# Another formula for the first feed-forward's activation: arctan, two squares and a cubic in place of a second tanh with correction steps

## The reference

```python
# attention: per head, state = f*state + k v^T, y = q.state, f = sigmoid(f_logit)   (4 x 8 heads, 768 steps, dim 48)
x = y as [3072 tokens, 384]
# first feed-forward, d_ff = 2048
h  = x @ w_in
sp = log1p(exp(h))                    # softplus
g  = h * tanh(sp)
x  = g @ w_out
# second feed-forward, d_ff = 1536
out = (sigmoid(x @ w_gate) * (x @ w_val)) @ w_out2
```

## Time and profile before

| what | value |
|---|---|
| median of 3 runs | 1093.04 us (1092.76 to 1094.50) |
| span of the profiled execution, first to last instruction | 1088.3 us |
| median less span: what lies around the instructions | 4.7 us |
| TensorE busy | 1023.6 us (94%) |
| VectorE busy | 671.0 us (62%) |
| ScalarE busy | 571.5 us (53%) |
| GpSimd busy | 137.2 us (13%) |
| mean granted TensorE clock | 0.989 |

### The profile page before, as it was taken

The page is one execution under the profiler, slowest core; times in us unless marked ns, Lnnn a source line. Parts: engine busy times, 40 slices in busy tenths (PEclk is TensorE's granted clock), DMA queues, the critical chain, the costliest instruction groups (busy, mean ns, idle before and its releaser), DMA issues.

```text
span 1088.3 us, 14401 instructions
## 1 busy us (share of the span) xinstructions
PE 1023.6 (94%) x4765; PEld 826.9 (76%) x4765; DVE 671.0 (62%) x1035; ACT 571.5 (53%) x1067; POOL 137.2 (13%) x147
## 2 busy tenths in 40 slices
PE   4999998899999999988898789999999999999997
PEld 3777777688887888876676668888888888888885
DVE  7999997699998999989999942222222222222221
ACT  5677775688887888876767632221222112321222
POOL 2222222500000000004554440000000000000000
PEclk9999999899999999999999999999999999999999
DMA  5544441200000000001111110000000000100001
GB/s 145 147 139 137 130 145 53 58 1 1 1 1 1 1 0 0 0 1 44 44 37 36 44 37 1 1 1 1 30 29 0 0 0 0 58 1 1 1 1 58
DMA packets 35345, 37.58 MB, mean 35 GB/s; under 512 B 4064, under 2 KB 26080, under 8 KB 35296
## 3 DMA queue, kind: packets, MB, share of 16 engines
q1 hardware_dynamic: 35296, 36.98, 11.3%
HBM read 32.24 MB, written 4.72 MB: 34 GB/s over the span
## 4 chain that ended last, share of the span: by engine, by line
PE 66%; DVE 23%; issue 5%; ACT 4%; DVEq 1%; DMA 0%; SPq 0%; ACTq 0%
PE bank L834 21%; PE bank L836 21%; PE bank L835 20%; DVE sets L697 3%; DVE sets L702 3%; DVE sets L699 3%; DVE glo L706 3%; DVE sets L690 2%; DVE sets L689 2%; DVE prefix L570 2%; ACT qt L410 1%; DVE probs L597 1%; PE bank L777 1%; PE bank L754 1%; DVE state L614 1%
## 5 line engine op out<-in xcount | busy, mean ns | idle before, releaser
L834 PE MATMUL bank<-xhi,whi 128*128 (+1 forms) x720 | 286.4, 398 | 5.3 <-ACT prod L515 3.7
L836 PE MATMUL bank<-xhi,wlo 128*128 (+1 forms) x720 | 284.5, 395 | 0.0
L835 PE MATMUL bank<-xlo,whi 128*128 (+1 forms) x720 | 282.7, 393 | 0.0
L734 DVE TENSOR_TENSOR prod<-prod,bank 128x512 f32<-128x512 f32 x72 | 49.5, 688 | 293.7 <-PE bank L836 292.7
L834 PE MATMUL bank<-ghi,whi 128*128 128x512 f32 x504 | 201.9, 401 | 29.0 <-DVE glo L706 28.8
L836 PE MATMUL bank<-ghi,wlo 128*128 128x512 f32 x504 | 199.0, 395 | 0.0
L835 PE MATMUL bank<-glo,whi 128*128 128x512 f32 x504 | 198.3, 393 | 0.0
L834 PEld LDWEIGHTS bank<-xhi,whi 128*128 128x128 f32 x720 | 136.4, 189 | 35.5 <-issue 4.4
L836 PEld LDWEIGHTS bank<-xhi,wlo 128*128 128x128 f32 x720 | 136.4, 189 | 32.2
L835 PEld LDWEIGHTS bank<-xlo,whi 128*128 128x128 f32 x720 | 136.6, 190 | 30.9
L515 ACT ACTIVATE prod<-bank 128x512 f32<-128x512 f32 x72 | 43.1, 598 | 189.6 <-PE bank L836 189.5
(11 more groups left out here) (75 smaller groups left out, 1269.9 us busy)
## 6 DMA issues: line engine op xcount, KB each, us to landing
raw<-w_out_dram SPq DMA_DIRECT2D x28, 192.0 KB, 2.4
xb<-f_dram SPq DMA_DIRECT2D x48, 96.0 KB, 2.4
kb<-k_dram SPq DMA_DIRECT2D x48, 96.0 KB, 2.2
qb<-q_dram SPq DMA_DIRECT2D x48, 96.0 KB, 2.2
vb<-v_dram SPq DMA_DIRECT2D x24, 192.0 KB, 2.4
out_dram<-rows_out SPq DMA_DIRECT2D x18, 256.0 KB, 2.1
raw<-w_in_dram SPq DMA_DIRECT2D x16, 192.0 KB, 2.7
raw<-w_gate_dram SPq DMA_DIRECT2D x12, 192.0 KB, 2.5
```

Of the source, the lines that this page charges most:

```text
L734: dve.tensor_tensor(prod[:, i % NSET], prod[:, i % NSET], h_ps[1][:, :], ALU.mult).then_inc(p_done, 1)
L834: pe.matmul(ps, hi, xh, start=first, stop=False)
L835: pe.matmul(ps, hi, xl, start=False, stop=False)
L836: return pe.matmul(ps, lo, xh, start=False, stop=last)
```

## The change

The activation is computed by another formula. With t = tanh(h/2), it takes a = arctan(0.5 - 0.5 t), y = (2·ROOT·a - ROOT·pi/4)², z = (y - Y_SHIFT)², and g = (MISH_K - (z + Z_SHIFT)·y)·(t + 1)·h. ScalarE does `start` (one tanh from PSUM), `angle` (arctan), `square`, `shifted` (a second square) and `high`: five instructions a unit. VectorE does `silu` ((t + 1)·h, which now reads `h` from PSUM and frees the bank), `cubic`, `finish` and `low`: four a unit. The semaphore that frees the PSUM bank is `silu_done` in place of `act_h`. The order of the functions within an iteration is another one on both engines.

```diff
-                act.activation(st[:, 0], h_ps[i % 2][:, :], ACT.Tanh, scale=0.5).then_inc(wsl_done, 1)
-                act.activation(st[:, 1], h_ps[i % 2][:, :], ACT.Silu).then_inc(act_h, 1)
+                act.activation(st[:, 0], h_ps[i % 2][:, :], ACT.Tanh, scale=0.5).then_inc(tanh_done, 1)

-            def seed(p, i):
-                act.wait_ge(wsl_done, p * N1 + i + 1)
-                act.activation(st[:, 2], st[:, 0], ACT.Square, scale=-0.5, bias=half_bias).then_inc(sqx_done, 1)
-                act.activation(st[:, 3], st[:, 0], ACT.Tanh, scale=0.5 * SEED_B, bias=seed_bias).then_inc(f0_done, 1)
-            def error2(p, i):
-                act.wait_ge(a_done, p * N1 + i + 1)
-                act.activation(st[:, 0], st[:, 2], ACT.Square, scale=-SEED_A, bias=one_bias).then_inc(sq_done, 1)
+            def angle(p, i):
+                act.wait_ge(tanh_done, p * N1 + i + 1)
+                act.activation(st[:, 2], st[:, 0], ACT.Arctan, scale=-0.5, bias=half_bias).then_inc(angle_done, 1)
+            def square(p, i):
+                act.wait_ge(angle_done, p * N1 + i + 1)
+                act.activation(st[:, 2], st[:, 2], ACT.Square, scale=2 * ROOT, bias=angle_bias).then_inc(square_done, 1)
+            def shifted(p, i):
+                act.wait_ge(square_done, p * N1 + i + 1)
+                act.activation(st[:, 3], st[:, 2], ACT.Square, bias=shift_bias).then_inc(shifted_done, 1)

-                for lag, do in ((2, high), (0, start), (1, error2), (0, seed)):
+                for lag, do in ((0, start), (1, square), (0, angle), (2, high), (1, shifted)):

-            def fold(p, i):
-                dve.wait_ge(f0_done, p * N1 + i + 1)
-                dve.scalar_tensor_tensor(st[:, 2], st[:, 2], 1.0, st[:, 3], ALU.add, ALU.mult).then_inc(y0_done, 1)
-                dve.scalar_tensor_tensor(st[:, 1], st[:, 0], 3.0, st[:, 1], ALU.subtract, ALU.mult).then_inc(a_done, 1)
+            def silu(p, i):
+                dve.wait_ge(tanh_done, p * N1 + i + 1)
+                dve.scalar_tensor_tensor(st[:, 1], st[:, 0], 1.0, h_ps[i % 2][:, :], ALU.add, ALU.mult).then_inc(silu_done, 1)
+            def cubic(p, i):
+                dve.wait_ge(shifted_done, p * N1 + i + 1)
+                dve.scalar_tensor_tensor(st[:, 3], st[:, 3], Z_SHIFT, st[:, 2], ALU.add, ALU.mult).then_inc(cubic_done, 1)
             def finish(p, i):
-                dve.wait_ge(a_done, at)
-                dve.scalar_tensor_tensor(st[:, 1], st[:, 2], 2.0 / SEED_A, st[:, 1], ALU.subtract, ALU.mult).then_inc(c_done, 1)
-                dve.wait_ge(sq_done, at)
-                dve.scalar_tensor_tensor(st[:, 3], st[:, 0], 1.0, st[:, 3], ALU.add, ALU.mult).then_inc(b_done, 1)
-                dve.wait_ge(c_done, at)
-                dve.wait_ge(b_done, at)
-                dve.scalar_tensor_tensor(st[:, 2], st[:, 1], SEED_A * SEED_A / 2, st[:, 3], ALU.mult, ALU.mult).then_inc(g_done, 1)
+                dve.wait_ge(silu_done, p * N1 + i + 1)
+                dve.wait_ge(cubic_done, p * N1 + i + 1)
+                op = dve.scalar_tensor_tensor(st[:, 1], st[:, 3], MISH_K, st[:, 1], ALU.subtract, ALU.mult, reverse0=True)
+                op.then_inc(g_done, 1)

-                for lag, do in ((2, low), (1, finish), (0, fold)):
+                for lag, do in ((0, silu), (1, cubic), (2, low), (1, finish)):

-                wait(pe, act_h, p * N1 + i - 1)
+                wait(pe, silu_done, p * N1 + i - 1)
```

More of the change, by code:

```diff
@@ L15 @@
+import math
 from contextlib import ExitStack
@@ L48 @@
 ZEROED = 12
-SEED_A, SEED_B, SEED_C = 1.388922696938513, 0.57335997, 0.36783547
+ROOT, Y_SHIFT, Z_SHIFT, MISH_K = 0.2798491220034162, 1.200595289745728, 0.8158012363459893, 0.6035533808434461
 def run(eng, count, n, lead, tail, step):
@@ L108, in attention_mlp_mlp @@
         guard_col, guard_min, safe_flag = consts[:, 6:7], consts[0:1, 9:10], consts[0:1, 10:11]
-        half_bias, one_bias, seed_bias = consts[:, 0:1], consts[:, 1:2], consts[:, 2:3]
+        half_bias, angle_bias, shift_bias = consts[:, 0:1], consts[:, 1:2], consts[:, 2:3]
         shared = top[0]
@@ L192, in attention_mlp_mlp @@
         w_hi_done, w_ready = sem("w_hi_done"), sem("w_ready")
-        h_done, act_h, wsl_done = sem("h_done"), sem("act_h"), sem("wsl_done")
-        f0_done, y0_done, a_done, sq_done = sem("f0_done"), sem("y0_done"), sem("a_done"), sem("sq_done")
-        b_done, c_done, g_done = sem("b_done"), sem("c_done"), sem("g_done")
+        h_done, tanh_done, silu_done = sem("h_done"), sem("tanh_done"), sem("silu_done")
+        angle_done, square_done, shifted_done = sem("angle_done"), sem("square_done"), sem("shifted_done")
+        cubic_done, g_done = sem("cubic_done"), sem("g_done")
         ghi_done, g_ready, acc_done = sem("ghi_done"), sem("g_ready"), sem("acc_done")
         x2hi_done, x2lo_done = sem("x2hi_done"), sem("x2lo_done")
-        sqx_done = sem("sqx_done")
         gate_done, val_done, sig_done, p_done = sem("gate_done"), sem("val_done"), sem("sig_done"), sem("p_done")
@@ L469, in start @@
                 wait(act, g_ready, p * N1 + i + 1 - reuse(i))
-                act.activation(st[:, 0], h_ps[i % 2][:, :], ACT.Tanh, scale=0.5).then_inc(wsl_done, 1)
-                act.activation(st[:, 1], h_ps[i % 2][:, :], ACT.Silu).then_inc(act_h, 1)
-            def seed(p, i):
+                act.activation(st[:, 0], h_ps[i % 2][:, :], ACT.Tanh, scale=0.5).then_inc(tanh_done, 1)
+            def angle(p, i):
                 st = sets[:, i % NSET]
-                act.wait_ge(wsl_done, p * N1 + i + 1)
-                act.activation(st[:, 2], st[:, 0], ACT.Square, scale=-0.5, bias=half_bias).then_inc(sqx_done, 1)
-                act.activation(st[:, 3], st[:, 0], ACT.Tanh, scale=0.5 * SEED_B, bias=seed_bias).then_inc(f0_done, 1)
-            def error2(p, i):
+                act.wait_ge(tanh_done, p * N1 + i + 1)
+                act.activation(st[:, 2], st[:, 0], ACT.Arctan, scale=-0.5, bias=half_bias).then_inc(angle_done, 1)
+            def square(p, i):
                 st = sets[:, i % NSET]
-                act.wait_ge(a_done, p * N1 + i + 1)
-                act.activation(st[:, 0], st[:, 2], ACT.Square, scale=-SEED_A, bias=one_bias).then_inc(sq_done, 1)
+                act.wait_ge(angle_done, p * N1 + i + 1)
+                act.activation(st[:, 2], st[:, 2], ACT.Square, scale=2 * ROOT, bias=angle_bias).then_inc(square_done, 1)
+            def shifted(p, i):
+                st = sets[:, i % NSET]
+                act.wait_ge(square_done, p * N1 + i + 1)
+                act.activation(st[:, 3], st[:, 2], ACT.Square, bias=shift_bias).then_inc(shifted_done, 1)
             def high(p, i):
@@ L488, in high @@
                 wait(act, acc_done, p * N1 + i - 1)
-                act.activation(ghi[:, i % 2], sets[:, i % NSET, 2], ACT.Copy).then_inc(ghi_done, 1)
+                act.activation(ghi[:, i % 2], sets[:, i % NSET, 1], ACT.Copy).then_inc(ghi_done, 1)
             def sums_high(p, i):
@@ L550, in _ @@
             dve.memset(consts[:, 0:1], 0.5).then_inc(zeroed, 1)
-            dve.memset(consts[:, 1:2], 1.0).then_inc(zeroed, 1)
-            dve.memset(consts[:, 2:3], 0.5 * SEED_B + SEED_C).then_inc(zeroed, 1)
+            dve.memset(consts[:, 1:2], -ROOT * math.pi / 4).then_inc(zeroed, 1)
+            dve.memset(consts[:, 2:3], -Y_SHIFT).then_inc(zeroed, 1)
             dve.memset(state[:, :, :], 0.0).then_inc(state_done, 1)
@@ L896, in mlp1 @@
                 if isinstance(p, int) and (p, i) == (NPASS, 0):
-                    pe.wait_ge(act_h, NPASS * N1)
+                    pe.wait_ge(silu_done, NPASS * N1)
                     gate_val(0, 0)
```

4 lines of the change are left out of this document (2 added, 2 removed).

## The result

| | before | changed |
|---|---|---|
| median, us | 1092.9 (4 runs, 1090.39 to 1094.50) | 1115.07 (4 runs, 1112.24 to 1116.13) |
| ratio | 1 | 1.0205, 95% interval 1.0184 to 1.0226 |
| span of the profiled execution, us | 1088.3 | 1110.4 |

The account below looks back on a forecast made before the run. TensorE was taken to bound 64 units and VectorE 32; +16 (passes one and two), +4.6 (turns), +4 (last pass) and -1.8 (table loads) made +23 on 1088.3, plus 4.7 around the span: 1116 us, range 1104 to 1127.

Parts of the forecast that it names:

- The new chain: From tanh to TensorE's project: low part reaches TensorE at 4.45 us, wanted at 3.95; 4.43 us a unit against 4.15.
- my signs: Trace marks of being right, such as TensorE waiting on L713 in nearly every unit and tanh spacing 4.4.
- Passes one and two: About 28 of 33 slots in each pass steady, each 0.28 us slower: +16 us.
- the turns: Between passes, accumulator copies ahead of ScalarE's iteration lengthen the chain to the low part: +2.3 us a turn, +4.6.
- The last pass: Cubic and low part fall under GpSimd's split: 5.0 us a unit against 4.84, +4 us over 28 units.
- Table loads: Two loads of 1283 ns go, at the first unit and before the second feed-forward: -1.8 us.
- The base of the sum: The 4.7 us that the median has around the profiled span, added to 1111 to give 1116 us.
- (A): VectorE is relieved and TensorE never kept waiting, the low part ready 0.5 us earlier: 1070 us, faster; 5%.
- (B): The stall under GpSimd mostly goes, last pass at 4.43 to 4.6 us a unit: 1100 us; 8%.
- (C): TensorE's clock falls after waits in every second pair of the last pass, 13 us more: 1129 us; 6%.
- (D): Arctan sits in another table than tanh, two loads a unit, 246 us: 1339 us; under 1%.
- My 5 us: Last pass, if VectorE's two loop instructions waited out GpSimd's under an exclusive port lock: 5 us more, 1121 us.

Follow-up runs that it names:

- low_before_cubic: Changed kernel with VectorE's low part moved ahead of the cubic in its order: 1062.79 us, ratio 0.9719 to the kernel before.
- the dose: Changed kernel with the cubic computed on only 256 of 512 columns: 1094.32 us; pace 4.30 us a unit in pass one.
- before_low_late: Kernel before (old formula) with VectorE's low part moved from first to last in the iteration: 1205.66 us.
- after_split_late: Changed kernel with GpSimd's split of the second feed-forward's weights begun only at the end of the last pass: 1096.25 us.
- high_last: Changed kernel with ScalarE's last two functions exchanged, shifted before high: 1081.6 us, ratio 0.9912 to the kernel before.

## Why the prediction was right

**The new chain.** Right in each link. Forecast from the start of the tanh: shifted at 2.25, cubic 3.01, low part 3.61, TensorE 4.45, two units in 8.86. Measured: 2.24, 2.99, 3.60, 4.43, and 4.42 a unit. Its cause is shown by low_before_cubic (pace 4.15 once the low part is freed) and by the dose; before_low_late shows only that a late low part costs time under the old formula too. Two things I did not have. The ring through the set (4.38 us a unit) is only 0.05 us shorter than mine, so by this working a chain some 0.1 us longer would have begun to be paid in full in each unit and not by halves. And of my signs, TensorE's waits on L713 in nearly every unit are not in the list of waits: they lie under the recorded durations, and show as the 0.4 us pauses of the weight queue.

**Passes one and two.** Forecast +16 us steady and +4.6 at the turns. From the first tanh of a pass to the first of the next it was 137.6 and 137.4 us, and is 147.6 and 147.1: +19.7 together. Steady: 28 x 0.275 = 7.7 each, 15.4. Idle at the turns: between the first tanh of pass one and the first of pass three the changed kernel has the waits at 334.93, 353.85 and 482.00, 6.86 us, and the old one 1.79 + 0.59 = 2.38, which is 4.5 more. Both terms stand, the sum being 0.2 us over the measured one.

**The last pass.** The pace was right (5.0 forecast, 4.98 measured), with its reason, cubic and low part under GpSimd, and 1.18 us of wait for a forecast of 1.3. The loop closes through TensorE as forecast, 9.96 us a pair for 9.99. The other tanh of the pair is held by the set, which I had not seen; by the spacings that costs nothing here, since the set alone would let the next one go at 550.47 + 4.38 = 554.85, just ahead of the 554.93 that TensorE gives it. But from its first to its last tanh the pass is only 1.4 us longer (150.5 to 151.9), not 4: the first five distances between tanh starts make 24.7 us in the old kernel and 22.6 in the changed one. The old kernel has four waits of TensorE there (1.79, 1.05, 0.60 and 0.54 us, at 480.30 to 495.70), the changed one a single one of 2.60. I had not priced that start.

**Table loads and the end of the stage.** Here a step failed. I gave -1.8 us for two loads. Both are gone, and TensorE's wait before the second feed-forward fell from 3.66 to 2.61 us; its first matmul there, before and changed:

```profile
636.78 0.73 PE L834 MATMUL bank<-xhi,whi 128*128 128x512 f32 x1 [3.66 <-ACT prod L515]
```
```profile
657.63 0.80 PE L841 MATMUL bank<-xhi,whi 128*128 128x512 f32 x1 [2.61 <-DVE xlo L721]
```

But from the last tanh to the end of the span the changed kernel is 2.3 us longer (468.1 to 470.4). 1.0 us of that lies ahead of these two matmuls (16.6 us from the last tanh, 17.6 changed), where the last units leave the ring; no run takes this part further. The other 1.3 lie behind them (451.5 and 452.8 us to the end of the span), and there the granted clock differs. Two windows of the changed kernel:

```profile
640.00:660.00 20.00, 15.26 (x60) 11.87 (x61) 12.26 (x17) 9.71 (x17) 9.77 (x12) 0.92 0.18 53
660.00:680.00 20.00, 20.00 (x81) 16.21 (x80) 4.42 (x7) 3.69 (x6) 4.56 (x6) 0.91 0.04 13
```

20 x 0.08 + 20 x 0.09 = 3.4 us lost at 1.2 GHz in place of 2.4. The clock was still full (1.00) from 640 to 650 us, where a wait of 2.06 us lies, and had fallen (0.85) from 650 to 660 us, with the one of 2.61; the kernel before lost 1.8 us at the same place, with its wait of 3.66. The time at half clock was longer in the changed kernel; why is open. This miss (+3.6 against a forecast of -1.3 for the second load) and the one in the last pass (-2.6) nearly cancel; the total is better than its parts, and that is luck. All parts together: -1.2 up to the first tanh (194.7 and 193.5), +19.7, +1.4, +2.3, which makes the 22.1 us between the spans but for rounding. Of the -1.2 about 0.8 lie ahead of the first matmul of this stage (190.35 and 189.57), where nothing is changed.

**The base of the sum.** I added 4.7 us for what lies around the span, the median less the span. The profiled executions are runs of 1090.39 and 1112.24 us with spans of 1088.3 and 1110.4: about 2 us lie around, and the rest was the spread of the runs. It did no harm, since it stands in both totals.

**The rivals.** (A) needed the low part 0.5 us earlier, and low_before_cubic gives it 1.2 us: there the kernel becomes what (A) described, with 1062.8 us for a forecast of 1070. (B), the last pass at 4.43, is what after_split_late shows when GpSimd is removed, and high_last half shows (4.57), though its chain is also half a microsecond shorter. (C): the last pass keeps clock 1.00 with its waits of 1.18 us. (D): no load but the attention's is in the trace.

**The port under GpSimd.** By the Trainium skill ("SBUF — State Buffer", "Who interferes with whom"), the pair of ports that VectorE and GpSimd share is an exclusive lock, and a VectorE instruction with two inputs in SBUF contends with a GpSimd instruction that reads SBUF; that one side fully blocks for the other's whole instruction it says of VectorE's modes with two ports. My 5 us took that over to these instructions. The rows here show VectorE's 1.51 us beside GpSimd's 1.02 and 0.97, both records running at once, and the pair's loss was what the rows of before gave (9.95 us a pair), not the 5 us more of that sum. The records cannot show whether an instruction that is on record is in truth held; the sum can be made without deciding it. The same section says that a VectorE instruction with at most one input in SBUF, outside the modes with two ports, does not contend; silu (L695), with its other input in PSUM, agrees: 0.68 us inside GpSimd's 1.35 at 546.11 in low_before_cubic, and 685 ns in the mean of 96.

## What to carry to other kernels

Before counting what a change removes, follow the one result that the bounding engine waits for through every queue it stands in, with start-to-start spacings, and compare its arrival with the time it is wanted: removing two of six instructions lost 22 us, and exchanging two entries of an ordering tuple then turned that into 30 us of gain. An urgent instruction whose input is ready must not stand behind one whose input comes last in the same iteration. Where three in-order engines wait in a ring, none is the bound, whatever the busy shares say (58, 67 and 99% here): count matmuls per stretch, and divide the ring's length by the number of units it carries. A result that two engines wait for, here the low part, closes two rings: work out both.

## What the runs showed of the hardware beyond the forecast

A stage at 99% TensorE busy did 6% fewer matmuls (410 for 436 in 100 us), since a pause of 0.2 us (0.45 from start to start, 303.52 to 303.97, for 0.23) vanishes under recorded durations. Under GpSimd's split, VectorE's fp32 instructions with two SBUF inputs take 1.5 us against its subtraction (0.69 alone). Where an instruction starts against GpSimd's decides whether it is lengthened: 0.69 us for the cubic that starts 0.22 us ahead of the subtraction (high_last), 1.51 for the one 0.05 us behind it (changed).
